# Where the last three groups of ahead-computed scores stand at the end of the first batch

## The chip, the core and the metric

The kernel runs on one core of a Trainium2 chip. The metric is the device time of one execution in microseconds (us); lower is better. The engines are TensorE (PE: matmuls and transposes; PEld its weight loads), VectorE (DVE), ScalarE (ACT), GpSimd (POOL) and SyncE (SP, which issues most DMAs). ScalarE issues some DMAs too.

## The reference

What is computed, cut to what matters here: attention with a top-32 mask over 4 batches, 8 heads, 576 tokens and head width 64, followed by a Fourier mixing of tokens and channels, and two MLP blocks of width 512 and 2048.

```python
scores = scale * np.matmul(q, k.transpose(0, 1, 3, 2))      # (4, 8, 576, 576)
kth = np.partition(scores, -32, axis=-1)[..., -32:-31]
scores = np.where(scores >= kth, scores, -1e9)
attn = softmax(scores)
x = (attn @ v) laid out as (4, 576, 512)
X = np.fft.fft(np.fft.fft(x, axis=1), axis=2)
u = x + np.real(X)
un = (u - mean) / sqrt(var + 1e-6)
x = u + np.maximum(un @ w_ch1, 0.0) @ w_ch2
x = x + np.maximum(norm(x) * g_ln @ w2_ch1, 0.0) @ w2_ch2
```

## The kernel before

**Tiles and slots.** The attention is cut into 144 tiles (`TILES`), 36 for each of the four batches (`NT`). A tile is 128 rows of scores of one head (two half-filled tiles stand for the remaining 64 tokens of a head pair). Each engine has its own program, written by hand as a loop over slots `s`; in slot `s` TensorE transposes the probabilities of tile `s` (`probs_T`), computes the scores of tile `s + 4` (`scores`), and, for each second tile, multiplies by the values (`values`) and transposes the result back (`values_back`). ScalarE copies the probabilities out (`probs_out`), copies the scores (`scores_out`), makes the exponentials (`exps`) and copies the result's transposes (`x_out`, `x_back`). VectorE works on pairs of tiles: four rounds of `max` and three of `match_replace` on each to find the 32nd largest score, and one masking (`scalar_tensor_tensor`, which is tensor `ex` in the rows).

**Scores ahead.** TensorE has room in the first batch, so the scores of the third and fourth batch (72 tiles, in 36 groups `e` of two tiles, `AHEAD`) are computed there. `scores_ahead(e)` fills all four banks of `Big` with one group; `scores_aside(e)` on ScalarE copies it into one of four buffers (two in a spare part of `U`, one in `un`, one in `yb`); `store_aside(e)`, a DMA issued by ScalarE's queue, sends it to `sc_ahead` in DRAM. `Big` holds one group only, so `scores_ahead(e)` waits until group `e - 1` is copied (`s_ah_sb`). Much later `scores_in` loads them back. Before the change, TensorE computes group `s - 1` at the end of slot `s`, for `s` from 1 to 36, and ScalarE copies group `s - 2` in slot `s`, between the probabilities' copy and the scores' copy, and stores it a little later in the same slot.

**The seam.** Slot 35 is the last of batch 0. When its result is copied (`x_back(35)`), VectorE may run `normal_x(0)`, `pair_x(0)` and `fold_x(0)`, which stand in its program behind the search for tiles 36 and 37. Slot 37 (`SEAM`) then runs all ten pieces of the first batch's transform (`dft_piece(0, i)`), which use the banks of `Big`: they wait for VectorE's last fold (`s_fold`) and until all 36 groups are copied (`s_ah_sb` at 36). The first MLP work begins in slot 39. VectorE's first normalisation waits for the store of group 34 (its buffer is `un`), the first result for that of group 35 (`yb`).

In the profile's rows, L669 is the products of a group (L663 for the half-filled tiles), L897 its copy, L901 its store; L684 `probs_T`, L642 `scores`, L706 `values`, L715 `values_back`, L927 `probs_out`, L886 `scores_out`, L943 `x_out`, L779 and L791 the transform's products, L958 their copies, L1140, L1146 and L1153 VectorE's search and masking, L1206 the last fold.

Of the kernel before, what the change touches and what calls it, by code (L numbers as in the profile page):

```python
# [37 lines left out]
WFS = 3  # L38
AHEAD = NT
ASIDE = 4  # L40
KEPT = TILES - 2 * AHEAD
SIDE = (B // 2) * NHP

# [23 lines left out]
def slot_of(n):  # L67

    return SLOT_OF[n]
# [15 lines left out]
def closing_at(s):  # L85

    if s == START[0]:
        return []
    return [n for n in range(NUNITS) if slot_of(n) == s - 1][-1:]


def turn_slot(t):
# [125 lines left out]
def build(nc, q, k, v, g2, w_raw, seq_t, wid_t, alt_t, w_low, sc_ahead, out):  # L218
# [4 lines left out]
    with ctx:  # L223
# [67 lines left out]
        s_ah_ps, s_ah_sb = sem("s_ah_ps"), sem("s_ah_sb")  # L291
        s_ah_st = [sem(f"s_ah_st{n}") for n in range(ASIDE)]
        s_ah_in = [sem("s_ah_in0"), sem("s_ah_in1")]
# [34 lines left out]
        def aside_buffer(e):  # L328

            if e % ASIDE < 2:  # L330
                return aside[:, e % ASIDE, :, :]
            free = un if e % ASIDE == 2 else yb
# [289 lines left out]
        def _(pe):  # L622
# [203 lines left out]
            for s in range(SLOTS):  # L826
# [30 lines left out]
                    values_back(s)  # L857
                for n in second_at(s):
                    mlp1(n)
                if 0 < s <= AHEAD:  # L860
                    scores_ahead(s - 1)
                if s == SEAM:
                    pe.wait_ge(s_tab, 48)
                    for b, i in pieces:
# [10 lines left out]
        def _(act):  # L875
# [23 lines left out]
            def store_aside(e):  # L899
                act.wait_ge(s_ah_sb, e + 1)  # L900
                nc.scalar.dma_start(sc_ahead[e], aside_buffer(e)).then_inc(s_ah_st[e % ASIDE], 16)  # L901
# [115 lines left out]
            def weights_high(j):  # L1017
                act.wait_ge(s_wraw[j % WFS], 16 * (j // WFS + 1))
                if j >= WRING:
                    act.wait_ge(s_wst[j % WRING], 16 * (j // WRING))  # L1020
                nc.scalar.activation(wr[:, j % WRING, :, 0, :], wf[:, j % WFS, :, :], ACT.Copy).then_inc(s_whigh, 1)
# [17 lines left out]
            for s in range(SLOTS):  # L1039
                pieces = [(b, i) for b in range(B) for i in range(PIECES) if piece_slot(b, i) == s]  # L1040
                if s < TILES:
                    probs_out(s)
                    if s == START[0]:
                        for t in turns_at(s):
                            un_out(t)
                    if 0 <= s - 2 < AHEAD:
                        scores_aside(s - 2)
                    if s + RING < KEPT:
                        if s not in SCORED.values():
                            scores_out(s + RING)  # L1050
                    elif s % 2 == 0 and s + RING < TILES:
                        scores_in((s + RING) // 2)
                    if s % 2 == 0 and s < 2 * KF:
                        weights_high(s + 1)
                    if 0 <= s - 2 < AHEAD:
                        store_aside(s - 2)
                    if s % 2 == 0 and s + 2 < TILES and s not in (START[0] - 3, START[0] - 1, START[0] + 1) and not late_exps(s):
                        exps(s + 2)
                        exps(s + 3)
                    if s % 2 == 1 and late_exps(s - 1):  # L1060
                        exps(s + 1)
                        exps(s + 2)
# [30 lines left out]
                            normalise(p, j)  # L1093
                if s % 2 == 1 and s + 1 < 2 * KF:
                    weights_high(s + 1)
                if s == SEAM:
                    exps(s + 1)
                    exps(s + 2)
                    for b, i in pieces:
                        piece_out(b, i)  # L1100
                        if i == 0:
                            high_1(0)
                        if i == 1:
                            high_2(0)
                            high_1(1)
                        if i == 2:
                            high_2(1)
                        if i == 3:
                            high_1(2)
# [277 lines left out]
```

## Time and profile before

| what | value |
|---|---|
| median of 3 runs | 1361.39 us |
| lowest and highest | 1359.71, 1363.40 us |
| the profiled execution | 1362.1 us |
| its span in the trace | 1360.3 us |
| mean granted TensorE clock in it | 0.977 of full |
| TensorE busy | 1252.0 us (92%) |
| VectorE busy | 1101.4 us (81%) |
| ScalarE busy | 798.4 us (59%) |
| GpSimd busy | 356.6 us (26%) |

The span is cut in 40 slices of 34 us; a digit gives the busy tenths of an engine in one of them. The chain of waits is followed back from the last instruction, so it shows the work that set the end. A time in a row is counted from the start of the span. A granted clock of 1.00 is 2.4 GHz, 0.50 is 1.2 GHz.

### The profile page before, as it was taken

To read this page: it belongs to the slowest core of one execution; us is meant where nothing else is said; L and a number is where in the kernel's file an instruction comes from. 1 tells how busy PE (TensorE), PEld (TensorE's weight loads), DVE (VectorE), ACT (ScalarE), POOL (GpSimd) and SP (SyncE) were. 2 spreads that over 40 slices of the span, in tenths; PEclk is the share of its full clock that TensorE was granted. 3 is DMA by queue.
4 is the path that set the end of the run, shared out by engine and by line. 5 is a ranking of instruction groups with operands and counts; after the bars stand their busy time and mean duration, and the time that the engine had idled before them with its cause. 6 is when DMAs were issued, how large, how long until landed. Compare 5 with 4: busy or idle time off the path is not lost.

```text
span 1360.3 us, 22775 instructions
## 1 busy us (share of the span) xinstructions
PE 1252.0 (92%) x7944; PEld 1024.3 (75%) x7944; DVE 1101.4 (81%) x2196; ACT 798.4 (59%) x1586; POOL 356.6 (26%) x327
## 2 busy tenths in 40 slices
PE   5776778999999899999988999999989999999999
PEld 3444444787777778788876888887679999999997
DVE  7999999899999989999999779975484454646453
ACT  4777765578777646776665557664353434343442
POOL 2444430122232431223335123333030111212110
PEclk9989978999999899999999999999999999999999
DMA  7899993567757757777885577753244343333342
GB/s 249 321 338 340 327 325 145 186 223 252 244 194 259 236 189 251 267 259 241 263 285 197 168 231 238 259 195 129 80 153 142 123 148 117 128 115 127 119 148 85
DMA packets 118259, 282.21 MB, mean 207 GB/s; under 512 B 29825, under 2 KB 29826, under 8 KB 118146
## 3 DMA queue, kind: packets, MB, share of 16 engines
q1 hardware_dynamic: 106386, 233.55, 51.7%
q10 hardware_dynamic: 10368, 42.47, 8.3%
q0 software_dynamic: 1392, 4.73, 1.1%
q8 instruction: 65, 1.06, 0.3%
q14 instruction: 48, 0.39, 0.1%
HBM read 237.44 MB, written 42.73 MB: 206 GB/s over the span
## 4 chain that ended last, share of the span: by engine, by line
PE 57%; DVE 36%; issue 5%; ACT 1%; POOL 1%; DMA 1%; SPq 0%; ACTq 0%; DVEq 0%
PE Big L752 23%; DVE top L1140 15%; PE Big L735 15%; DVE wk L1146 14%; PE Sp L735 7%; DVE ex L1153 3%; PE Tp L684 3%; PE Sp L779 2%; PE Tp L706 2%; PE Sp L791 1%; DVE st L1232 1%; PE Tp L811 1%; PE Big L779 1%; PE Sp L642 1%; PE Big L791 0%
## 5 line engine op out<-in xcount | busy, mean ns | idle before, releaser
L752 PE MATMUL Big<-wr,hh 128*128 128x512 f32 x1152 | 361.4, 395 | 0.0
L735 PE MATMUL Big<-uh,wr 128*128 128x256 f32 (+1 forms) x1400 | 320.9, 319 | 7.1 <-ACT hh L990 6.8
L1140 DVE MAX8 top<-wk 128x8 f32<-128x576 f32 x432 | 304.3, 745 | 0.0
L735 PEld LDWEIGHTS Big<-uh,wr 128*128 128x128 f32 x1400 | 236.5, 191 | 26.3 <-issue 16.5
L752 PEld LDWEIGHTS Big<-wr,hh 128*128 128x128 f32 x1152 | 217.6, 189 | 41.1
L752 PE MATMUL Big<-wr,hl 128*128 128x512 f32 x576 | 238.7, 414 | 4.8 <-DVE wr L1285 4.6
L512 POOL TENSOR_TENSOR hl<-hf,hh 128x256 fp32r<-128x256 f32 (+1 forms) x126 | 108.5, 861 | 452.5 <-ACT hh L990 452.5
L735 PE MATMUL Big<-ul,wr 128*128 128x256 f32 (+1 forms) x700 | 218.6, 312 | 0.0
L1146 DVE MATCH_REPLACE8 wk<-top,wk 128x576 f32<-128x576 f32 x288 | 211.4, 741 | 0.0
L684 PE MATMUL Tp<-ident,ex 128*128 128x128 f32 x720 | 117.1, 289 | 47.2 <-DVE ex L1153 38.3
L927 ACT ACTIVATE pT<-Tp 128x640 f32<-128x640 f32 x144 | 101.1, 702 | 88.1 <-PE Tp L684 87.9
L684 PEld LDWEIGHTS Tp<-ident,ex 128*128 128x128 f32 x720 | 86.5, 146 | 87.6 <-issue 50.8
L990 ACT ACTIVATE hh<-Big 128x384 fp32r<-128x384 f32 (+1 forms) x175 | 75.5, 432 | 118.1 <-PE Big L735 118.1
L1153 DVE SCALAR_TENSOR_TENSOR ex<-sc,top,ex 128x576 f32<-128x576 f32 x144 | 124.6, 902 | 18.8 <-ACT ex L920 18.7
L752 PEld LDWEIGHTS Big<-wr,hl 128*128 128x128 f32 x576 | 108.5, 188 | 34.8 <-issue 15.7
L735 PEld LDWEIGHTS Big<-ul,wr 128*128 128x128 f32 x700 | 133.5, 191 | 0.0
L1140 DVE MAX8 top<-sc 128x8 f32<-128x576 f32 x144 | 101.6, 746 | 16.6 <-ACT sc L886 9.5
L1146 DVE MATCH_REPLACE8 wk<-top,sc 128x576 f32<-128x576 f32 x144 | 105.7, 741 | 0.0
L920 ACT ACTIVATE ex<-sc,nmx 128x576 f32<-128x576 f32 x144 | 104.0, 769 | 2.3
L506 POOL TENSOR_TENSOR wr<-wf,wr 128x1024 fp32r<-128x1024 f32 x32 | 75.3, 2368 | 111.3 <-DVE top L1140 109.3
L989 ACT ACTIVATE hf<-Big 128x256 f32<-128x256 f32 (+1 forms) x126 | 52.2, 414 | 82.0 <-PE Big L735 82.0
L706 PE MATMUL Tp<-pT,vn 128*64 128x128 f32 x1280 | 87.9, 286 | 12.4 <-ACT pT L927 11.9
(136 smaller groups left out, 1832.1 us busy)
## 6 DMA issues: line engine op xcount, KB each, us to landing
wf<-in_weights SPq DMA_DIRECT2D x208, 512.0 KB, 3.6
wr<-w_low SPq DMA_DIRECT2D x252, 256.0 KB, 4.3
sc<-in_weights SPq DMA_DIRECT2D x48, 512.0 KB, 3.2
sc<-sc_ahead ACTq DMA_DIRECT2D x36, 576.0 KB, 5.6
w_low<-wr SPq DMA_DIRECT2D x32, 512.0 KB, 6.6
sc_ahead<-U ACTq DMA_DIRECT2D x18, 576.0 KB, 5.2
sc_ahead<-un ACTq DMA_DIRECT2D x9, 576.0 KB, 4.1
sc_ahead<-yb ACTq DMA_DIRECT2D x9, 576.0 KB, 6.5
```

The costliest lines, as they stand in the source:

```text
L506: pool.tensor_tensor(wr[:, r, :, 1, :], wf[:, j % WFS, :, :], wr[:, r, :, 0, :].bitcast(f32), ALU.subtract).then_inc(s_wlow, 1)
L512: pool.tensor_tensor(hl[:, n % 2, 0:w], hf[:, n % 2, 0:w], hh[:, n % 2, 0:w].bitcast(f32), ALU.subtract).then_inc(s_hl[0], 1)
L684: last = nc.tensor.transpose(Tp[:, c * P:(c + 1) * P], ex[:, s % RING, c * P:(c + 1) * P], ident[:, :])
L706: last = nc.tensor.matmul(OT[h * D:(h + 1) * D, :], vn[:, par, c, h, 0:D], pT[:, h, c * P:(c + 1) * P], start=(c == 0), stop=(c == C - 1))
L735: last = nc.tensor.matmul(hidden(n), a[:, kd * P:(kd + 1) * P], x[:, kd, 0:P * SIZE[p]], start=(kd == 0 and j == 0), stop=(kd == KD - 1 an ...
L752: last = nc.tensor.matmul(Ac[:, j, :], a[:, n % 2, j * P:(j + 1) * P], w, start=(f == 0 and m == 0), stop=(f == KF - 1 and m == 2))
L920: nc.scalar.activation(ex[:, s % RING, 0:S], sc[:, s % RING, :], ACT.Exp, bias=nmx[:, s % RING:s % RING + 1], scale=1.0 / np.sqrt(D)).then ...
L927: nc.scalar.activation(pT[:, s % 2, :], Tp[:, 0:C * P], ACT.Copy).then_inc(s_pT_sb, 1)
L990: nc.scalar.activation(hh[:, n % 2, 0:w], hidden(n), ACT.Relu).then_inc(s_h_sb, 1)
L1140: nc.vector.max(top[:, s % RING, r, :], src).then_inc(s_top, 1)
L1146: nc.vector.match_replace(out=wk[:, a, :], in_to_replace=top[:, s % RING, r, :], in_values=src, imm_value=STRUCK).then_inc(s_struck, 1)
L1153: nc.vector.scalar_tensor_tensor(out=ex[:, s % RING, 0:S], in0=sc[:, s % RING, :], scalar=top[:, s % RING, ROUNDS - 1, 7:8], in1=ex[:, s % ...
```

## The change

`made_at(s)` now says which groups TensorE computes at the end of slot `s`: group `s - 1` for slots 1 to 33, none in slot 34, groups 33, 34 and 35 in slot 35, none in slot 36. `taken_behind(s)` says which groups ScalarE copies and stores, one after the other, near the end of slot `s`: group 32 in slot 33, and groups 33, 34, 35 in slot 35, behind `x_back(35)`. For groups 0 to 31 nothing changes. The work is the same; only its place differs.

```diff
+LAST = AHEAD - 1
+def made_at(s):
+
+    if s == LAST:
+        return [LAST - 2, LAST - 1, LAST]
+    return [s - 1] if 0 < s < LAST - 1 else []
+
+
+def taken_behind(s):
+
+    return {LAST - 2: [LAST - 3], LAST: [LAST - 2, LAST - 1, LAST]}.get(s, [])
...
-                if 0 < s <= AHEAD:
-                    scores_ahead(s - 1)
+                for e in made_at(s):
+                    scores_ahead(e)
...
-                    if 0 <= s - 2 < AHEAD:
+                    if 0 <= s - 2 < LAST - 3:
                         scores_aside(s - 2)
...
-                    if 0 <= s - 2 < AHEAD:
+                    if 0 <= s - 2 < LAST - 3:
                         store_aside(s - 2)
...
+                for e in taken_behind(s):
+                    scores_aside(e)
+                    store_aside(e)
```

TensorE's program from slot 34's transposes to the transform (`Big<-U` is a group, `Tp<-ident,ex` the transposes of a tile's probabilities), before:

```order
140 L684 MATMUL Tp<-ident,ex 128x128 x5
141 L642 MATMUL Sp<-kT,qT 128x288 x2
142 L669 MATMUL Big<-U 128x288 x4
143 L684 MATMUL Tp<-ident,ex 128x128 x5
144 L642 MATMUL Sp<-kT,qT 128x288 x2
145 L706 MATMUL Tp<-pT,vn 64x128 x10
146 L715 MATMUL Tp<-ident,xT 128x128
147 L669 MATMUL Big<-U 128x288 x4
148 L684 MATMUL Tp<-ident,ex 128x128 x5
149 L642 MATMUL Sp<-kT,qT 128x288 x2
150 L669 MATMUL Big<-U 128x288 x4
151 L684 MATMUL Tp<-ident,ex 128x128 x5
```

and now:

```order
140 L697 MATMUL Tp<-ident,ex 128x128 x5
141 L655 MATMUL Sp<-kT,qT 128x288 x2
142 L697 MATMUL Tp<-ident,ex 128x128 x5
143 L655 MATMUL Sp<-kT,qT 128x288 x2
144 L719 MATMUL Tp<-pT,vn 64x128 x10
145 L728 MATMUL Tp<-ident,xT 128x128
146 L682 MATMUL Big<-U 128x288 x12
147 L697 MATMUL Tp<-ident,ex 128x128 x5
148 L655 MATMUL Sp<-kT,qT 128x288 x2
149 L697 MATMUL Tp<-ident,ex 128x128 x5
```

Groups 33, 34 and 35 stood at the ends of slots 34, 35 and 36, and stand together behind the result's transpose (`Tp<-ident,xT`) of slot 35.

ScalarE's program from slot 35's probabilities to the first result copy behind slot 37, before:

```order
247 L927 ACTIVATE pT<-Tp 128x640 [waits s_pv_ps,s_pT_ps]
248 L897 ACTIVATE U<-Big 128x2x2x288 [waits s_ah_st1,s_ah_ps]
249 L886 ACTIVATE sc<-Sp 128x2x288 [waits s_masked,s_sc_ps]
250 L901 DMA sc_ahead<-U 128x1152 [waits s_ah_sb]
251 L943 ACTIVATE xT<-Tp 128x128 [waits s_xb_ps,s_pv_ps]
252 L951 ACTIVATE U<-Tp 128x128 [waits s_xb_ps]
253 L927 ACTIVATE pT<-Tp 128x640 [waits s_pv_ps,s_pT_ps]
254 L897 ACTIVATE un<-Big 128x2x2x288 [waits s_ah_st2,s_ah_ps]
255 L886 ACTIVATE sc<-Sp 128x2x288 [waits s_masked,s_sc_ps]
256 L901 DMA sc_ahead<-un 128x1152 [waits s_ah_sb]
257 L927 ACTIVATE pT<-Tp 128x640 [waits s_pv_ps,s_pT_ps]
258 L897 ACTIVATE yb<-Big 128x2x2x288 [waits s_ah_st3,s_ah_ps]
```

and now:

```order
247 L940 ACTIVATE pT<-Tp 128x640 [waits s_pv_ps,s_pT_ps]
248 L899 ACTIVATE sc<-Sp 128x2x288 [waits s_masked,s_sc_ps]
249 L956 ACTIVATE xT<-Tp 128x128 [waits s_xb_ps,s_pv_ps]
250 L964 ACTIVATE U<-Tp 128x128 [waits s_xb_ps]
251 L910 ACTIVATE U<-Big 128x2x2x288 [waits s_ah_st1,s_ah_ps]
252 L914 DMA sc_ahead<-U 128x1152 [waits s_ah_sb]
253 L910 ACTIVATE un<-Big 128x2x2x288 [waits s_ah_st2,s_ah_ps]
254 L914 DMA sc_ahead<-un 128x1152 [waits s_ah_sb]
255 L910 ACTIVATE yb<-Big 128x2x2x288 [waits s_ah_st3,s_ah_ps]
256 L914 DMA sc_ahead<-yb 128x1152 [waits s_ah_sb]
257 L940 ACTIVATE pT<-Tp 128x640 [waits s_pv_ps,s_pT_ps]
258 L899 ACTIVATE sc<-Sp 128x2x288 [waits s_masked,s_sc_ps]
```

The copies (`<-Big`) and their stores left slots 35, 36 and 37 and stand in a row, each store right behind its copy.

## Rows read from the trace of the kernel before

**Rows 1.** The page: the span, and busy tenths in 40 slices.

```profile
span 1360.3 us, 22775 instructions
...
PE   5776778999999899999988999999989999999999
...
DVE  7999999899999989999999779975484454646453
...
PEclk9989978999999899999999999999999999999999
```

**Rows 2.** The chain of waits, 200 to 250 us: start, length, engine and what.

```profile
216.17 0.73 DVE top L1140 x2
...
218.37 1.12 PE Tp L684 x5
...
220.11 1.14 ACT un L897
221.29 2.29 PE Big L669 x8
223.58 1.26 PE Tp L684 x5
224.84 0.98 PE Sp L642 x4
225.83 1.27 PE Tp L706 x20
```

**Rows 3.** Timeline of slots 33 to 35: start, length, instructions, idle before.

```profile
205.73 1.24 PE L669 MATMUL Big<-U 64*128 64x288 f32 x8
...
208.63 1.13 ACT L897 ACTIVATE U<-Big 128x1152 f32<-128x1152 f32 x1
209.64 0.66 ACT L886 ACTIVATE sc<-Sp 128x576 f32<-128x576 f32 x1
...
214.30 0.33 PE L715 MATMUL Tp<-ident,xT 128*128 128x128 f32 x1 [0.45 <-ACT xT L943]
...
214.55 1.24 PE L669 MATMUL Big<-U 64*128 64x288 f32 x8
...
221.27 0.33 ACTq L901 DMA_DIRECT2D sc_ahead<-un  x1
```

**Rows 4.** TensorE: stretches (length, busy, granted clock, DMA), and its timeline at 196.

```profile
190.00:194.00 4.00, 2.54 (x29) 1.00 0.79 308
194.00:198.00 4.00, 1.90 (x13) 1.00 0.71 230
198.25:201.25 3.00, 2.56 (x12) 0.50 0.91 307
208.00:212.00 4.00, 2.87 (x19) 1.00 0.37 151
212.00:216.00 4.00, 3.24 (x33) 1.00 0.37 149
216.00:218.00 2.00, 0.00 (x0) 1.00 0.00 0
219.00:221.00 2.00, 1.74 (x7) 0.50 0.03 8
...
226.00:228.00 2.00, 1.62 (x23) 1.00 0.27 111
...
196.14 0.74 PE L684 MATMUL Tp<-ident,ex 128*128 128x128 f32 x5 [1.66 <-DVE ex L1153]
196.80 0.76 PE L642 MATMUL Sp<-kT,qT 64*128 64x288 f32 x4
```

**Rows 5.** Timeline of slots 36 and 37 and the transform's start.

```profile
219.41 1.33 PE L642 MATMUL Sp<-kT,qT 64*128 64x288 f32 x4
...
226.21 0.67 DVE L1206 TENSOR_TENSOR xf<-xs 128x510 f32<-128x510 f32 x1
...
227.61 4.72 PE L779 MATMUL Big<-seq,xf 128*128 128x320 f32 x14
```

## The prediction

> **What bounds the kernel now.** I read the page first [rows 1]: VectorE is 90% or more busy in most slices up to about the 23rd, TensorE is the fuller engine behind that, and the granted clock shows a few slices below full. The change touches only the end of the first batch, some 25 us around 205 to 228 us, so the next view is the chain of waits there [rows 2]. It runs on VectorE until the search of the pair of tiles 36 and 37 ends, goes over to TensorE at 218.37 us with the transposes of tile 36, and then goes through just the work that is moved: the copy of group 34 (ScalarE, 1.14 us), the products of group 35 (2.29), the transposes and scores of slot 37 (1.26, 0.98), its values (1.27), and into the transform of batch 0 at 227.61. The transform's pieces follow one another on TensorE from there, and the chain stays with them. What is won or lost at 227.61 is therefore won or lost at the end, as long as no other chain is close behind.
>
> One is close. The transform also waits for VectorE's last fold, which ends at 226.21 + 0.67 = 226.88 us [rows 5]. VectorE is busy without a break from the search of tiles 36 and 37 to that fold, and nothing of its work is moved. So the transform can't start before about 226.88 + 0.04 = 226.92 (0.04 being the step from the copy's end, 220.11 + 1.14, to TensorE at 221.29 [rows 2]). **The most that this change can give is 227.61 - 226.92 = 0.69 us.** That is the reason why I exclude a larger gain.
>
> **Part 1, slots 33 to 35.** Before, group 32 is computed at 205.73 (1.24 us) and copied at 208.63, behind the probabilities of tile 34; now its copy and its store stand at the end of slot 33. The copy starts at about 206.97 + 0.04 = 207.01, lasts 1.13 and ends at 208.14; the store's issue takes 0.33 [rows 3] and can't start before the copy is done, so the probabilities' copy of slot 34 starts at 208.5; before it stood ahead of the copy of 208.63 and, by its own 0.6, started at 208.0: 0.5 later. In return ScalarE has no 1.13 us copy before the scores' copy of that slot, which moves from 209.64 to about 209.15, and with it the exponentials behind it and the probabilities of tile 35. With them the values of tile 35 come 0.5 earlier, and the place where the row of three begins, behind the transpose of the result at 214.30, comes at 214.05 instead of 214.55 [rows 3]. Group 33 also left TensorE between slots 34 and 35. Gain so far 0.5 us; the bounds are 0 (the store's issue holds ScalarE longer than its row says) and 0.7.
>
> **Part 2, the row of three.** The Big banks hold one group, so the three groups alternate strictly: products, copy, products, copy. This is the added wait: the second and third group wait on TensorE for ScalarE, and queued behind them on TensorE stand the transposes of tile 36. At the full clock one round is 1.24 (products) + 1.13 (copy) + 2 x 0.04 = 2.45 us; a store's issue of 0.33 fits beside the next products of 1.24 and costs nothing. Two rounds and one more set of products from 214.05 end at 214.05 + 4.90 + 1.24 = 220.19. Up to 218.37 TensorE had nothing else to do before: it is empty from 215.8 on, with 0.00 of 2 us busy from 216 to 218 [rows 4], so the part up to 218.37 is covered by the search on VectorE. The rest, 220.19 - 218.37 = 1.82 us, is not: tile 36's transposes wait for it.
>
> The clock decides how long it lasts. Before, TensorE's granted clock is at 0.50 (1.2 GHz) from 219 on, right behind that empty stretch, and at 1.00 (2.4 GHz) again from 226 [rows 4]. The groups of this kind show the price: 1.24 us at the high level [rows 3] and 2.29 at the low one [rows 2]. The new row has no empty stretch of 2.5 us, but two pauses of 1.21 between the groups. The nearest row I find is 194 to 198, where TensorE is busy 1.90 of 4 us with a pause of 1.66, and the clock is at 0.50 right behind it; in the new row it is busy 1.24 of each 2.45 us. A denser stretch before it (2.54 of 4) was at the full clock and left it there [rows 4]. So I take it that the clock falls here too, at about the old place: the third group, from 218.95, then takes 2.29 and ends at 221.24; its copy ends at 222.41 and its store is issued by 222.8.
>
> **Part 3, slots 36 and 37.** They lose two sets of products (group 35 alone cost 2.29) and two copies of 1.13. Tile 36's transposes run from 221.28 and, at the low level, take 1.26 (as tile 37's do before), with scores of 1.33 behind them, to 223.9 [rows 2, 5]. ScalarE's copy of these probabilities runs beside the scores, from 222.8 to 223.5. Tile 37's transposes begin at 223.9. From there to the transform stand the same steps as before, 227.61 - 223.58 = 4.03 us [rows 2, 5]. That gives a transform at 227.9: **+0.3 us**. If the clock comes back at about 222 instead of shortly before 226 (it did after the fall at 198, where about three us were at the low level and 2.56 of the 3 us were busy at 0.50 [rows 4]), transposes and scores take 0.74 and 0.76 [rows 4], tile 37's transposes wait only for the probabilities' copy until 223.55, and the steps from there shrink by 1.26 - 0.74 and 0.98 - 0.76 to 3.29: 226.8, which is the fold's bound of 226.92 within 0.1. I write 227.0: **-0.6 us**.
>
> **What follows.** The transform lasts the same; the store of group 34 leaves at about 219, before its old 221.27 [rows 3], that of group 35 by 222.8, and their buffers un and yb are next needed by the normalisation and the first result behind the transform. SyncE's and GpSimd's queues have none of the moved work in them and nothing is moved past theirs. The loads of q and k for later batches wait for groups up to the 27th only. I add nothing for these.
>
> **The sum.** Part 1 and 2 and 3 end between -0.6 and +0.3 us, middle about -0.15, of which I keep 0.1. The profiled execution is 1362.1 us (span 1360.3 [rows 1] and 1.8 around it), 0.7 above the median of the runs shown; on the median that makes 1361.4 - 0.1 = 1361.3 us.
>
> **The rivals.**
> *The clock stays high.* The new row breaks the only empty stretch of that place, 215.8 to 218.37. Then the row ends at 220.19, tile 36's transposes and scores by 221.7, the last copy with its store by 221.8, the probabilities' copy by 222.5, and the remaining 3.29 us are over at 225.8, before the fold: the transform starts at 226.92. Time: 1361.4 - 0.7 = 1360.7. For it speaks that the longest pause falls from 2.5 to 1.2 us; against it the fall behind 194 to 198 [rows 4]. The Trainium skill (TensorE: Matmul & The Clock Gate, "Why this matters for your kernels") advises to avoid long idle gaps between bursts of matmuls; by that rule this rival would hold, and the row at 194 to 198 does not agree with it.
>
> *Slower: the low clock holds through the whole row.* The place is slots 34 and 35, where TensorE loses group 33 between two tiles and so becomes emptier just before the row. If the clock falls before the row begins, three sets of products take 2.29 and the copies with their steps 1.21: 214.05 + 3 x 2.29 + 2 x 1.21 = 223.34 for the last products, 225.9 behind tile 36's transposes and scores at 1.26 + 1.33, then 4.03: transform at 230.0, **+2.4 us**. The transform's first fourteen products take 4.72 us at the full clock [rows 5]; if they run at the low level this is paid twice, up to **+7.1**. Time: 1363.8 to 1368.5, about 1365 the likeliest. It decides against the change from the point where 1.7 us of the transform's work are paid twice: then it passes 4.1 us. Against it: the stretch 208 to 216 was at 1.00 with 2.87 and 3.24 of 4 us busy [rows 4], and the row ends in unbroken work of the last group, tile 36's transposes and its scores, 4.9 us at the low level. The Trainium skill (the same page, "A second HAM failure mode: psum-queue depth-cycling") says that short idles between groups of matmuls, as they wait for their banks, are enough to make the clock swing; that speaks against this change, and by it the fall comes in the row of three rather than never.
>
> *It is absorbed.* Another chain is as late as the transform, and a shift of half a us either way is gone by 250 us. For it speaks that VectorE's fold is only 0.69 us ahead; against it that the chain stays on TensorE through the transform, whose work can't start earlier than its first piece. Time 1361.4.
>
> That the change doesn't do what it says is no rival: the order of both engines shows the three groups in one row.
>
> **How the numbers follow.** The forecast (-0.6 to +0.3) has 0.62, the high clock 0.18, the low clock 0.13, absorbed 0.04, and 0.03 is left for a gain or loss downstream that I can't name. 0.3%, about what a measurement of this kernel can tell from no change, is 4.1 us. Only the upper half of the slower rival and part of the rest pass it: slower 0.07, faster 0.02, within 0.91. The three runs of before lie 3.7 us apart (1359.71 to 1363.4), so I put 1.9 us around the outer ends of the first two cases, and reach into the lower part of the slower one, which starts at 1363.8: 1360.7 - 1.9 = 1358.8 to 1364.4.
>
> **What would show it.** In the profile after: group 32 copied at about 207 us; three sets of products with copies between them from about 214; the granted clock at 0.50 in that row or right behind it; tile 36's transposes at 220.2 to 221.3; the fold's end unmoved at 226.9, and the transform between 226.9 and 227.9. I am wrong if the transform starts after 229, if the three groups start later than 214.6, or if the time moves by more than 2 us with the transform in its place.

## The result and the profile after

| | before | after |
|---|---|---|
| median | 1359.86 us (20 runs) | 1363.03 us (20 runs) |
| lowest and highest | 1358.16, 1363.40 us | 1360.12, 1367.26 us |
| the profiled execution | 1362.1 us | 1360.17 us |

The ratio is 1.0021 with a 95% interval of 1.0013 to 1.0028: the change costs 2.9 us (1.8 to 3.8). The forecast was -0.1 us. The profiled execution of the changed kernel happens to be among its fastest, and that of before among its slower ones: from the start of the transform's second half (TensorE's first products with `wid`) to the end, before takes 1122.2 us and the changed kernel 1119.4, though none of that work is changed. So the two spans can't be compared; the seam inside them can.

The page of the changed kernel (span, busy tenths in 40 slices, answers to [rows 1]):

```profile
span 1358.4 us, 22775 instructions
...
PE   5777778999999899899988999999989999999999
...
DVE  7999999899999989999999779875484454646453
...
PEclk7978998999999999999989999999999999999999
```

Little differs: VectorE's digits are nearly those of before, and the slices with a lowered clock lie in part elsewhere. The chain of waits of the changed kernel (start, length, engine, what) answers to [rows 2]. Lines are 13 higher than in before up to VectorE's part: L682 is a group's products, L910 its copy, L697 tile transposes, L940 the copy of the probabilities, L719 values, L792 the transform.

```profile
212.63 1.34 PE Tp L719 x20
...
214.65 1.20 PE Big L682 x8
215.87 1.14 ACT U L910
217.05 2.07 PE Big L682 x8
219.15 1.14 ACT un L910
220.33 2.32 PE Big L682 x8
222.67 1.14 ACT yb L910
224.26 0.71 ACT pT L940
225.02 0.79 PE Tp L697 x5
...
228.68 4.56 PE Big L792 x14
```

Before, the chain stayed on VectorE until 218.37 [rows 2]. Now it has left VectorE by slot 34 and runs through the whole row of three: products, copy, products, copy, products, copy. The second products take 2.07 us and the third 2.32; the granted clock is 1.00 from 214 to 217 and 0.50 from 218 to 224 (TensorE: length, busy, granted clock, DMA share, GB/s):

```profile
214.00:217.00 3.00, 1.50 (x9) 1.00 0.00 0
218.00:224.00 6.00, 4.78 (x21) 0.50 0.47 188
225.00:228.00 3.00, 2.77 (x29) 1.00 0.36 147
```

The transform begins at 228.52 us, 1.74 behind the end of VectorE's last fold at 226.78. Before it was 227.61 and 226.88, so 0.73 behind [rows 5]. That is 1.0 of the 2.9 us. The rest is not in this execution, which is why more profiles were taken. From here on, "the distance" is the time from the end of VectorE's last fold to the start of the transform.

### The profile page after: what moved, and what is told of

It reads as the page before. It is cut to its first block, busy times and chain, and to the rows that moved or that the text cites. A ratio compares the mean times of both kernels' runs of the same rounds, so it can differ in the third digit from the quotient of the medians.

```text
span 1358.4 us, 22775 instructions
## 1 busy us (share of the span) xinstructions
PE 1251.5 (92%) x7944; PEld 1023.5 (75%) x7944; DVE 1101.0 (81%) x2196; ACT 799.9 (59%) x1586; POOL 356.8 (26%) x327
## 4 chain that ended last, share of the span: by engine, by line
PE 57%; DVE 33%; issue 5%; POOL 2%; ACT 2%; DMA 1%; ACTq 0%; SPq 0%; DVEq 0%; POOLq 0%
PE Big L765 23%; PE Big L748 15%; DVE top L1156 14%; DVE wk L1162 13%; PE Sp L748 7%; DVE ex L1169 3%; PE Tp L697 2%; PE Sp L792 2%; PE Tp L719 2%; PE Sp L804 1%; PE Tp L824 1%; DVE st L1248 1%; PE Big L792 1%; PE Sp L655 1%; DMA sc<-sc_ahead 0%
## 5 line engine op out<-in xcount | busy, mean ns | idle before, releaser
L765 PEld LDWEIGHTS Big<-wr,hh 128*128 128x128 f32 x1152 | 217.2, 189 | 41.0
L697 PE MATMUL Tp<-ident,ex 128*128 128x128 f32 x720 | 119.5, 294 | 46.8 <-DVE ex L1169 38.0
L697 PEld LDWEIGHTS Tp<-ident,ex 128*128 128x128 f32 x720 | 88.2, 148 | 88.6 <-issue 50.7
L940 ACT ACTIVATE pT<-Tp 128x640 f32<-128x640 f32 x144 | 101.3, 703 | 82.0 <-PE Tp L697 81.8
L748 PE MATMUL Sp<-uh,wr 128*128 128x384 f32 (+1 forms) x392 | 96.5, 330 | 0.0
```

The costliest lines, as they stand in the source:

```text
L697: last = nc.tensor.transpose(Tp[:, c * P:(c + 1) * P], ex[:, s % RING, c * P:(c + 1) * P], ident[:, :])
L748: last = nc.tensor.matmul(hidden(n), a[:, kd * P:(kd + 1) * P], x[:, kd, 0:P * SIZE[p]], start=(kd == 0 and j == 0), stop=(kd == KD - 1 an ...
L765: last = nc.tensor.matmul(Ac[:, j, :], a[:, n % 2, j * P:(j + 1) * P], w, start=(f == 0 and m == 0), stop=(f == KF - 1 and m == 2))
L940: nc.scalar.activation(pT[:, s % 2, :], Tp[:, 0:C * P], ACT.Copy).then_inc(s_pT_sb, 1)
```

## Experiments

In these edits `fill(k)` is `k` transposes of the identity by TensorE, into columns that nobody reads, about 0.14 us each at the full clock: work with no use but to keep TensorE from standing empty. Theory 1 was that the row's length holds tile 36's transposes and so the transform; theory 2 that the loss lies behind the transform. Theories 3 and 4 were formed on the way.

**The kernel before, once more** (no edit).

> The kernel before once more, unchanged: the ratio shows what a measurement can tell, and its profile is a second execution of the seam. All theories expect 1.000 within 0.001. The transform started 0.73 us behind the end of VectorE's last fold in the first profile (227.61 against 226.88); if that distance depends on where the low clock falls, it differs here, between 0.1 and about 3 us; if it doesn't, it is 0.7 again.

Measured: 0.9999 (0.9988 to 1.0009), transform 0.92 us behind the fold. A measurement of five rounds tells about 0.001, and the distance was nearly that of the first profile.

**The changed kernel, once more** (no edit).

> The changed kernel once more: expected 1.001 to 1.003 of before. In its first profile the transform started 1.74 us behind the end of the last fold (228.52 against 226.78), though that execution was among its fastest (1360.17 us against a median of 1363.03). Theory 1 (the row of three, with the low clock falling into it at various places, holds tile 36's transposes): this execution shows another distance, 1.7 to 6 us, and the longer the more of the row is at 0.50. Theory 2 (the loss lies elsewhere, behind the transform): the distance is near 1.7 again and the rest of the span is longer.

Measured: 1.0018 (1.0007 to 1.0028), and a distance of 4.18 us. The whole row stood at the low clock here. TensorE's timeline:

```profile
212.73 2.40 PE L719 MATMUL Tp<-pT,vn 128*64 128x128 f32 x20 [1.24 <-ACT pT L940]
...
215.92 2.29 PE L682 MATMUL Big<-U 64*128 64x288 f32 x8
219.44 2.29 PE L682 MATMUL Big<-U 64*128 64x288 f32 x8 [1.23 <-ACT U L910]
222.96 2.29 PE L682 MATMUL Big<-U 64*128 64x288 f32 x8 [1.23 <-ACT un L910]
225.18 1.24 PE L697 MATMUL Tp<-ident,ex 128*128 128x128 f32 x5
...
231.14 4.73 PE L792 MATMUL Big<-seq,xf 128*128 128x320 f32 x14
```

Tile 35's values, 1.31 us at the full clock, already take 2.40; a round of the row takes 219.44 - 215.92 = 3.52 us. This is the prediction's slower rival with its price of a round (2.29 + 1.21 = 3.50), and the place is slots 34 and 35, as it said. Theory 1 holds so far: from the start of the transform's second half (241.66 us) to the end of the span it is 1119.3 us, as in the changed kernel's first profile (1119.4).

**A row of two.** Group 33 stays in slot 34:

```diff
-        return [LAST - 2, LAST - 1, LAST]
-    return [s - 1] if 0 < s < LAST - 1 else []
+        return [LAST - 1, LAST]
+    return [s - 1] if 0 < s < LAST else []
...
-    return {LAST - 2: [LAST - 3], LAST: [LAST - 2, LAST - 1, LAST]}.get(s, [])
+    return {LAST: [LAST - 1, LAST]}.get(s, [])
...
-                    if 0 <= s - 2 < LAST - 3:
+                    if 0 <= s - 2 < LAST - 1:
```

> Group 33 stays at the end of slot 34, as in the kernel before; only groups 34 and 35 stand together behind slot 35's transpose, and leave together. At the full clock the second group's products end at 214.55 + 2.45 + 1.24 = 218.24 us, before tile 36's transposes may start at 218.37, so no round of the row is uncovered, and TensorE's empty stretch of 2.5 us is half filled. Theory 1: the transform starts at or near the fold's bound, 0.1 to 0.7 us behind it; time 0.998 to 1.000 of before, 3 to 4 us under the changed kernel. Theory 2: 1.001 to 1.003, as the changed kernel.

Measured: 1.0048 (1.0026 to 1.0069), executions from 1360.65 to 1374.57. Theory 1 expected a gain and got the worst kernel of all, though the transform starts at its bound, as theory 1 said (0.10 us behind the fold; the row of two itself ran at 1.00). What is slow is the transform. TensorE's timeline, and its stretches before and in the transform:

```profile
227.10 8.99 PE L792 MATMUL Big<-seq,xf 128*128 128x320 f32 x14 [1.96 <-issue]
```

```profile
225.20:227.00 1.80, 0.00 (x0) 1.00 0.00 0
227.25:229.25 2.00, 2.00 (x4) 0.50 0.00 0
232.00:236.00 4.00, 4.00 (x7) 0.50 0.00 0
238.00:240.00 2.00, 2.00 (x7) 1.00 0.94 337
```

TensorE was ready 1.96 us early, stood empty, and the clock was at 0.50 when the fold let the transform go: its first fourteen products take 8.99 us instead of 4.72 [rows 5]. So theory 3, at this point a guess from one profile: what counts is where the low clock falls against the serial work from tile 36 through the transform, and standing empty right ahead of that work puts it there. **A second profile of the same kernel** was taken for that.

> A second profile of the row of two without fillers. Theory 3: the transform begins 0.05 to 0.3 us behind the fold's end, and its first fourteen products take 4.7 us (full clock) or up to 9 (low clock in them), by which the execution's time goes: about 1360 to 1363 or 1366 to 1374.

Measured: the transform 0.11 us behind the fold after a pause of 2.02 us, again 0.50 from 227.25 on, and 15.53 us from the fold's end to the transform's second half where a transform at the full clock takes 10.7. Its time was 1363.47 us: the dear transform was there, but the sum came lower than the 1366 to 1374 expected for it. The first profile was 4.15 us slower (1367.62), and that difference lies behind the seam: there the clock was at 0.50 once more in the last batch's transform, from 954 to 961 us, and from the first transform's second half to the end it took 1123.3 us against 1119.2. The executions above 1370 have something more that no profile caught.

**The row of three with its pauses filled.**

```diff
+                    if e in (LAST - 2, LAST - 1):
+                        fill(7)
```

> The changed kernel with seven extra transposes of the identity (0.14 us each, about 1.0 us, into unused columns of a scores bank) in each of the two pauses of the row of three; the output is the same. If the low clock is the cause (theory 1 in its clock form), the clock stays at 1.00 in the row, the products take 1.24 each, and the transform starts at the fold's bound: 0.998 to 0.999 of before. If the length of the row at any clock is the cause, the filling gains nothing: 1.001 to 1.003. If the clock falls all the same, the fillers take 0.28 each and the row is 1.8 us longer: 1.003 to 1.004.

Measured: 1.0015 (1.0003 to 1.0026), no gain to speak of. But the profile is no test of a row at the full clock: the clock had fallen before the row (granted 0.85 from 210 to 214, 0.50 from 214 to 218), the first products took 2.29, and only behind the first fillers did the others take 1.24. The transform was 2.68 us behind the fold. The low stretch ended at 219.6, 1.1 us after the first fillers began. It had lasted 7 us, as in the kernel before, so it isn't shown that the fillers ended it; what they may have done is keep it from going on to 226, as in the second profile of the changed kernel. This was also the slowest of the twelve executions (1365.10 us), with the low clock in the last transform too.

**The row of two, filled**, in the pause and ahead of the transform (TensorE waits there until group 35 is copied, as the transform does anyway):

```diff
+                    if e == LAST - 1:
+                        fill(7)
...
+                    pe.wait_ge(s_ah_sb, AHEAD)
+                    fill(12, Hp[:, 0:P])
```

> Groups 34 and 35 in a row of two, with extra transposes of the identity of about 0.14 us each: seven in the pause between the two groups and twelve (about 1.7 us) in the place where TensorE stood empty for 1.96 us before the transform; the output is the same. Theory 3 (formed after the row of two was slower, 1.0048: what counts is where the low clock falls, and TensorE standing empty right before the serial work puts it there; in that profile the transform began at its bound, 227.10, but its first fourteen products took 8.99 us instead of 4.72): the transform begins at 227.1 and runs at 1.00; 0.997 to 0.999 of before, and the runs spread less than the 14 us of the unfilled row of two. If the clock in the transform was chance: 1.002 to 1.007 as the unfilled one.

Measured: 0.9999 (0.9989 to 1.0008), executions from 1358.27 to 1363.07. Against the same kernel without fillers that is 6.8 us off the median and 11.5 off the highest, for extra work, and the two intervals are far apart. Its transform (TensorE's timeline) and the same stretches as above:

```profile
224.39 1.47 PE L688 MATMUL Big<-ident 128*128 128x128 f32 x12
227.17 4.82 PE L796 MATMUL Big<-seq,xf 128*128 128x320 f32 x14 [1.31 <-DVE xf L1230]
```

```profile
225.20:227.00 1.80, 0.66 (x7) 1.00 0.00 0
227.25:229.25 2.00, 2.00 (x7) 1.00 0.00 0
```

This is the test of theory 3, and it held, save that 0.997 to 0.999 was too much: it only reaches the time of before. The row ran at 1.00 without fillers too, so it will be the twelve ahead of the transform that matter, but the two fillings were not tried one at a time.

**The kernel before with its empty stretch filled** (behind group 34, slot 35):

```diff
+                if s == AHEAD - 1:
+                    fill(16)
```

> The kernel before with sixteen extra transposes of the identity (about 2.2 us) behind group 34 in slot 35, where TensorE has nothing to do until tile 36's probabilities are masked (0.00 of 2 us busy from 216 to 218). Theory 3: the clock stays at 1.00 there, group 35 takes 1.24 us instead of 2.29, the transform begins at the fold's bound, 0.7 us earlier: 0.9985 to 0.9995 of before. But TensorE then stands empty for up to a us before the transform, and if that draws the low clock into it, 1.000 to 1.003. If the fillers delay tile 36's transposes: 1.000.

Measured: 1.0001 (0.9982 to 1.0020); ten of eleven executions from 1358.29 to 1362.81, one at 1373.56. In the profile group 35 takes 1.24 us and the transform begins 0.11 us behind the fold at 1.00, so the seam is 0.6 better. The ratio shows no gain, where 0.9985 to 0.9995 was expected. The kernel leaves a pause of 1.23 us ahead of the transform. The one far execution would fit a low clock in the transform, but it was not profiled.

**Group 32's copy and store alone moved.**

```diff
-    if s == LAST:
-        return [LAST - 2, LAST - 1, LAST]
-    return [s - 1] if 0 < s < LAST - 1 else []
+    return [s - 1] if 0 < s <= AHEAD else []
...
-    return {LAST - 2: [LAST - 3], LAST: [LAST - 2, LAST - 1, LAST]}.get(s, [])
+    return {LAST - 2: [LAST - 3]}.get(s, [])
...
-                    if 0 <= s - 2 < LAST - 3:
+                    if 0 <= s - 2 < AHEAD and s - 2 != LAST - 3:
```

> Only part 1 of the change: group 32's copy and store stand at the end of slot 33; groups 33 to 35 stay as in the kernel before. The sum of the prediction had this at -0.5 to 0 us. All theories: 0.999 to 1.001. If the loss of the change sat in this part (ScalarE held before tile 34's probabilities), it would be 1.001 to 1.003.

Measured: 1.0004 (0.9995 to 1.0013), distance 0.99. This part costs no more than 0.0013.

**The three groups left out.**

```diff
-        return [LAST - 2, LAST - 1, LAST]
+        return []
...
-    return {LAST - 2: [LAST - 3], LAST: [LAST - 2, LAST - 1, LAST]}.get(s, [])
+    return {LAST - 2: [LAST - 3], LAST: []}.get(s, [])
...
-                        pe.wait_ge(s_ah_sb, AHEAD)
+                        pe.wait_ge(s_ah_sb, AHEAD - 3)
...
-                nc.scalar.dma_start(sc[:, first:first + 2, :], sc_ahead[e]).then_inc(s_ah_in[e % 2], 16)
+                nc.scalar.dma_start(sc[:, first:first + 2, :], sc_ahead[min(e, AHEAD - 4)]).then_inc(s_ah_in[e % 2], 16)
```

> The changed kernel without groups 33, 34 and 35: their products, copies and stores are left out, and group 32's scores are loaded in their place later. So all the work that the change moves is gone. Theory 1 (the length of the row costs): the transform begins at the fold's bound and the kernel is 1 to 4 us faster than before, 0.997 to 0.9995. Theory 3 (emptiness costs): the transform begins at the bound, but TensorE is emptier than in any other kernel ahead of it, the low clock falls into the transform in many executions, and the kernel is no faster than before or slower, 1.000 to 1.005, with a wide spread.

Measured: 1.0001 (0.9987 to 1.0016), from 1358.16 to 1368.46. With the three moved groups gone, nothing is gained. Its profile, of one of the slower executions (1365.66 us), shows the low clock from 206.6 to 223.8 us, 1.00 for three us, a pause of 1.36, and then the transform at the low clock:

```profile
226.81 8.03 PE L793 MATMUL Big<-seq,xf 128*128 128x320 f32 x14 [1.36 <-issue]
```

**The row of three filled in all places** (beside the seven in each pause, eight in slot 34 and twelve ahead of the transform, the latter by the lines shown for the row of two):

```diff
+                if s == LAST - 1:
+                    pe.wait_ge(s_ah_sb, LAST - 2)
+                    fill(8, Hp[:, 0:P])
```

> The changed kernel with extra transposes of the identity in four places: eight in slot 34, where group 33 stood before (in the second profile of the changed kernel and in that of the row with filled pauses, the clock had fallen by 213 us, before the row), seven in each pause of the row, twelve before the transform. The output is the same. Theory 3: the clock stays at 1.00 from 206 us to the transform's end, the row takes 6.2 us, tile 36's transposes come about 1.8 us late and that is still covered by VectorE's fold: transform 0.05 to 0.1 us behind the fold's end, 0.999 to 1.0005 of before, 2 to 3 us under the changed kernel. If the serial row itself costs, at any clock: 1.0015 to 1.003.

Measured: 1.0004 (0.9994 to 1.0013). The clock was at 1.00 from 206 to 238 us and the row's products at 1.24 each. The transform was still 1.60 us behind the fold, but by my own edit: TensorE was ready at about 227.0 and then had twelve fillers (1.47 us) to run, which this kernel didn't need. Even so it is 2.4 us under the changed kernel's median, with the same row of three and more work on TensorE. That is the strongest evidence that the low clock is most of the loss, though the two intervals touch (0.9994 to 1.0013 against 1.0013 to 1.0028). That the row alone, at the full clock, would begin the transform at 0.05 to 0.1 us behind the fold failed: without the last twelve fillers TensorE was ready 0.3 us behind it.

**Both the seam and the last transform filled.** Near 945 us TensorE waits 2.50 us for the last batch's fold, and the low clock falls into that batch's transform in some executions.

```diff
+                if (b, i) == (B - 1, 0):
+                    pe.wait_ge(s_pc_sb, PIECES * b)
+                    fill(15, Sp[:, 1, SO:SO + P])
...
+                if s == AHEAD - 1:
+                    fill(16)
```

> The kernel before with extra transposes of the identity in two places: sixteen behind group 34 in slot 35, and fifteen where TensorE waits 2.50 us for the last batch's fold, ahead of that batch's transform, near 945 us. In the profiles the first six products of that transform take 2.08 or 3.72 us, by whether the low clock falls into them, and the spans from the first transform's start to the end are about 1130 or about 1133 to 1134. Theory 3: the second filling takes the upper of the two groups of times away: median 1357.5 to 1359, 0.998 to 0.9992 of before, no execution over 1361. If the two groups of times have another cause: 1.000.

Measured: 1.0009 (0.9988 to 1.0030). Nine of twelve executions lie between 1358.47 and 1360.51, three between 1370.02 and 1370.30. "No execution over 1361" failed: this kernel too leaves 1.23 us ahead of the first transform empty. With that pause left open, 4 of 23 executions (this kernel and the one before with its empty stretch filled) lie above 1370; in the three measurements of the row of two with fillers ahead of the transform, none of 33 lies above 1363.1. None of the four was profiled, so that their clock was low in the transform is inferred.

**Two more profiles of the changed kernel.**

> A third profile of the changed kernel, for where the low clock falls in the row of three. So far the transform began 1.74 and 4.18 us behind the fold's end (before: 0.73 and 0.92). Theory 3: between 1 and 4.5 us again, and the larger the more of the three products take 2.29 us. A distance of 0.1, as with the clock at 1.00 throughout, would be the rare case.

> A fourth profile of the changed kernel: transform 0.7 to 4.5 us behind the fold's end (so far 1.74, 4.18, 0.73).

Measured: distances of 0.73 and 2.46 us, times 1361.24 and 1361.20. In the first the clock stayed at 1.00 through the whole row and all products took 1.24 us: the prediction's rival of the high clock. It brought no gain over before (its distance is that of before's first profile), and its ScalarE shows why part 1 of the sum was wrong:

```profile
207.07 0.28 ACT L964 ACTIVATE U<-Tp 128x128 f32<-128x128 f32 x1 [0.48 <-PE Tp L728]
...
208.19 1.13 ACT L910 ACTIVATE U<-Big 128x1152 f32<-128x1152 f32 x1 [0.84 <-PE Big L682]
...
209.35 0.33 ACTq L914 DMA_DIRECT2D sc_ahead<-U  x1
...
210.06 0.70 ACT L940 ACTIVATE pT<-Tp 128x640 f32<-128x640 f32 x1 [0.74 <-ACT U L910]
```

Slot 34's copy of the probabilities waits for group 32's products (0.84 idle), its copy, and 0.74 us around the store, where the sum had 0.36 (208.14 to 208.5). The store's own row accounts for 0.33; what holds ScalarE for the rest isn't shown.

**The kernel before, third profile.**

> A third profile of the kernel before: transform 0.7 to 1.0 us behind the fold's end (so far 0.73 and 0.92), the clock falling in the empty stretch near 218.

Measured: 1.35 us, above the range I gave.

**The row of three alone**, group 32 left in its old place:

```diff
-    return {LAST - 2: [LAST - 3], LAST: [LAST - 2, LAST - 1, LAST]}.get(s, [])
+    return {LAST: [LAST - 2, LAST - 1, LAST]}.get(s, [])
...
-                    if 0 <= s - 2 < LAST - 3:
+                    if 0 <= s - 2 < LAST - 2:
```

> The row of three alone: group 32 is copied and stored in slot 34, where it was before; groups 33 to 35 stand together as in the changed kernel. Theory 4 (part 1 of the sum has the wrong sign: in the changed kernel ScalarE waits 0.84 us for group 32's products, copies, and is idle 0.74 us around the store before it takes tile 34's probabilities, so the row begins at 214.6 to 215.9 instead of 214.4 to 214.6): the row begins at 213.6 to 214.1, and where the clock stays at 1.00 the transform is at the fold's bound; 1.000 to 1.001 of before, 1 to 2.5 us under the changed kernel. If the row is all of the loss: 1.0018 as the changed kernel.

Measured: 1.0025 (1.0014 to 1.0036). Theory 4 fell: as far as the intervals tell, the row is all of the loss. The row began at 215.35, not at 213.6 to 214.1, and the profile, at the full clock from slot 34 through the first transform, shows the transform 0.57 us behind the fold.

**The row of two and the last transform, filled**, and the same again, and the last transform alone in the kernel before. The edits are those shown above.

> The row of two with its fillers (0.9999 alone, executions from 1358.3 to 1363.1) and, in addition, fifteen extra transposes of the identity ahead of the last batch's transform, where TensorE waits 2.50 us. Theory 3: the seam and the last transform both run at 1.00, all executions lie between 1357.5 and 1360.5, median 1358.5 to 1359.2, 0.9985 to 0.9993 of before. If fillers only shift the low clock elsewhere: 1.000.

> The row of two with fillers in the seam and ahead of the last transform once more (0.9987, interval 0.9979 to 0.9996). If the gain is real: 0.998 to 0.9995 again, and again no execution above 1361.

> The kernel before with the fifteen extra transposes ahead of the last transform only; the seam is untouched. Theory 3: the last transform's first six products take 2.08 us; the share of executions with them at the low clock (3.72 us) goes, some 0.5 us of the median: 0.999 to 1.000. If all of the gain of the kernel with both sits here: 0.998 to 0.9992; if none: 1.000.

Measured: 0.9987 (0.9979 to 0.9996), median 1358.78; again 0.9987 (0.9978 to 0.9996), median 1358.60; and 0.9993 (0.9984 to 1.0002) for the last transform alone, whose median (1360.35 against 1360.15 for before beside it) shows no gain at all. The first two are the only kernels measurably faster than before, by 1.8 us, and their 22 executions lie between 1358.12 and 1360.44. TensorE's timeline in the seam and at the last transform:

```profile
224.66 1.47 PE L688 MATMUL Big<-ident 128*128 128x128 f32 x12
227.00 4.82 PE L799 MATMUL Big<-seq,xf 128*128 128x320 f32 x14 [0.86 <-DVE xf L1233]
...
944.73 1.80 PE L688 MATMUL Sp<-ident 128*128 128x128 f32 x15
947.40 2.08 PE L799 MATMUL Sp<-seq,xf 128*128 128x320 f32 x6 [0.88 <-DVE xf L1233]
```

In the row-only kernel, without fillers, the last of these was

```profile
948.77 3.72 PE L792 MATMUL Sp<-seq,xf 128*128 128x320 f32 x6 [2.51 <-DVE xf L1222]
```

How the gain splits between seam and last transform is not shown: the interval of 0.9993 overlaps that of 0.9987 and holds 1.000.

All twenty profiles of the seam, in us. The fold's end is at 226.7 to 227.1 in all. The low stretch is where the granted clock reads under 1.00 from slot 34 to the transform, read in steps of 0.2 us:

| kernel | low clock | transform behind the fold | second half behind the fold |
|---|---|---|---|
| before | 218.4 to 225.6 | 0.73 | 11.25 |
| last transform filled alone | 218.6 to 225.6 | 0.76 | 11.28 |
| before | 219.2 to 226.2 | 0.92 | 11.44 |
| group 32's copy alone moved | 219.4 to 226.4 | 0.99 | 11.51 |
| before | 220.4 to 227.4 | 1.35 | 11.87 |
| before with its empty stretch filled, two profiles | none | 0.11, 0.10 | 10.70, 10.69 |
| changed | none | 0.73 | 11.25 |
| changed | 207.0 to 210.6, 217.2 to 224.2 | 1.74 | 12.26 |
| changed | 218.2 to 225.2 | 2.46 | 12.98 |
| changed | 212.4 to 226.2 | 4.18 | 14.70 |
| row of three alone | none | 0.57 | 11.09 |
| row of three, pauses filled | 212.6 to 219.6 | 2.68 | 13.20 |
| row of three, filled in all places | none | 1.60 | 12.11 |
| row of two, two profiles | 227.0 to 237.4 in both | 0.10, 0.11 | 15.52, 15.53 |
| three groups left out | 206.6 to 223.8, 227.0 to 234.0 | 0.10 | 13.93 |
| row of two, filled, three profiles | none | 0.05, 0.06, 0.05 | 10.67, 10.67, 10.66 |

In the five profiles whose seam is that of before or nearly so, the distance rises with the start of the low stretch: the later the clock falls, the more of it lies in the work right ahead of the transform. With the stretch filled it is 0.1. The row of three is at 0.57 and 0.73 without any low clock, and higher with it.

## Why the prediction was wrong

**The frame was right.** The bound by VectorE's fold held in all profiles: no transform began less than 0.05 us behind it, and the prices of single steps were good (rounds of 2.47 at the full clock and 3.52 at the low one, forecast 2.45 and 3.50; transform at its bound 226.8 to 227.2, forecast 226.92). The chain moved onto the row as described, and the time, 1363.03, is near the range's upper part. What failed is the sum, which forecast a gain of 0.1 where 2.9 us are lost.

**The steps that failed, in the sum's own terms.** The first profile of the changed kernel is the case that the forecast reckoned with: the clock falls in the row and comes back before the transform. For an early return the sum had 223.55 + 3.29 = 226.84 us; the transform came at 228.52, 1.68 later. The row began 0.53 later than the 214.05 of part 1. The second group's products were at the low level too (2.06 us, not 1.24), which with the steps between makes 0.85. And from the row's end to the transform it took 5.90 us where the sum had 5.60, of which 0.21 lie in the last steps: from tile 37's transposes to the transform the sum shrank before's 4.03 to 3.29, and all four profiles show 3.50.

**Part 1 had the wrong sign.** It gave the row a start 0.5 us earlier, at 214.05, and named 0 as its lower bound. Counted from tile 34's transposes to the row's first products, before takes 214.55 - 207.25 = 7.30 us (7.30 and 7.32 in its other two profiles), the changed kernel 215.46 - 208.07 = 7.39 in the profile at the full clock (7.42 and 7.39 in two others, 8.57 in the one with the low clock ahead of the row), and the row-only kernel 215.35 - 208.13 = 7.22. So taking group 33 away gains 0.1 and moving group 32 costs about 0.2 (7.45 where it alone was moved). The step that failed is that the scores' copy of slot 34 moves from 209.64 to about 209.15, "and with it the exponentials behind it and the probabilities of tile 35". Counted from tile 34's transposes, that copy starts at 2.59 us in the changed kernel, 2.39 in before, and 1.90 by the sum: group 32's copy starts 0.12 behind these transposes, where I placed it 0.24 ahead of them, and ScalarE stands idle for 0.74 us around the store, not 0.36.

Part 1 isn't all that the rival of the high clock missed. That case had its condition in one profile and not its time: by its sum the last steps end at 225.8, 1.1 us ahead of the fold, and they ended at 227.53. Of these 1.7 us, 0.6 are part 1, 0.3 the steps behind the row, and 0.8 come from ahead of the change: tile 34's transposes began at 208.07 there, at 207.25 in the profile that the sum was made from, and at 208.00 in before's third profile. The fold's end didn't move with them. The sum took one execution's place of slot 34 against the fold for a fixed one.

**The clock was read as one place.** "So I take it that the clock falls here too, at about the old place" made a rule of one execution, and put only the third group at the low level. In four profiles of the changed kernel the clock was low from the second products on (1.74 and 2.46), from before the row (4.18), or not at all (0.73). In before the row of waits is short and most of it is covered by VectorE's search, so the same wandering costs 0.73 to 1.35. The row of three hasn't this cover: it leaves no slack before tile 36's transposes even at the full clock (1.82 us uncovered by the sum; in the profile they start at 221.57, about 3.3 after VectorE's masking would let them), and each us of low clock lengthens it. The distance rose from 1.0 in the mean of three profiles to 2.3 in the mean of four.

**The slower rival** had the right mechanism and place with a chance of 0.13; one profile in four showed it, at +4.18 - 0.73 = 3.5 us, inside its 2.4 to 7.1, though with the transform at full clock, where its sum gave 2.4. Its dearer end, the transform at the low clock, came in kernels that finish early, which I had not thought of: I took an early finish for free, since "The most that this change can give is 227.61 - 226.92 = 0.69 us" seemed to have no opposite. The quoted rule on short idles (the Trainium skill, TensorE: Matmul & The Clock Gate, "A second HAM failure mode: psum-queue depth-cycling") agrees with two of the four profiles, where the clock fell inside the row (from 217.2 and 218.2 us); in the third it had fallen at 212.4, ahead of the row, and the one at 1.00 speaks against it. The Trainium skill's rule against long gaps (the same page, "Why this matters for your kernels") would not have warned of the row of two: pauses of 1.96 and 2.02 us are shorter than the gaps it names, and 0.50 followed both times.

**The absorbed case** fell: from the transform's second half to the end it is 1119.3 to 1119.5 us in three of the four profiles of the changed kernel, with distances from 1.74 to 4.18.

**What stays open.** The profiles' mean difference at the seam is 1.3 us, of 2.9 measured on twenty executions. The four profiled executions of the changed kernel (1360.17 to 1362.77 us, mean 1361.35) lie below the median of 1363.03, three of them in the lowest quarter, so the dearer ones (up to 1367 us) were not seen; whether they are dearer by the seam or by something behind it isn't shown. That filling the row and what surrounds it takes away 2.4 of the 2.9 us speaks for the seam.

From the transform's second half to the end the spans vary by themselves, and two more places with a wait and a low clock go with it. Near 460 us TensorE waits 2.5 to 3 us for ScalarE. In twelve profiles the rest of the span takes 1118.5 to 1119.6 us. In the five where the clock then stayed low from 460 to 468, about twice as long as in most others, it takes 1120.9 to 1122.3; the two highest of these also have the low clock in the last transform (3.72 us against 2.08). In the three where the low clock stayed on in the last transform, for 7 us, it takes 1123.2 to 1123.3. The executions above 1370 in three kernels were never profiled.

## What to carry to other kernels

Price a move by where it leaves an engine waiting as much as by what it moves: work put in a row that alternates with another engine through one buffer needs cover for its whole length, at the slow price of its steps. Finishing early ahead of a long serial stage on TensorE can cost more than finishing just in time, if the engine then stands empty; a few useless transposes there can be worth their place. Where one profile shows a low clock, take several before its place goes into a sum.

## What the runs showed of the hardware

A pause of 1.96 to 2.02 us ahead of the transform was followed by about 10 us at 0.50 of TensorE's clock in both profiles of the row of two, with TensorE busy throughout, and cost 4.8 us (15.5 against 10.7 us behind the fold). In the filled kernels a pause of 0.86 to 1.31 us was followed by 1.00. The pause's length doesn't decide it alone: with the three groups left out, a pause of 1.36 us was followed by 0.50. In the row of two, filling the pause ahead of the transform with transposes of the identity, 0.14 us each, went with 1.00 in all three profiles. Where the clock falls differs between executions of one kernel: in the changed kernel from 212.4, 217.2 or 218.2 us, or not at all. Leaving out three of 36 groups of products did not make the kernel faster (1.0001). With a DMA issued by ScalarE right behind the copy that it sends, the engine stood idle for 0.74 us in slot 34 and for 0.46 in the row, though the issue's own row reads 0.33.
